# Output product of the later tiles: four of its twelve chunks as three products of rounded parts

## The reference

```python
# 1: attention, 8 heads of 64; only the 32 largest scores of each row count
scores = scale * q @ k.T;  scores[scores < kth] = -1e9
x = softmax(scores) @ v                                  # -> (1152, 512)
# 2: a gated block of width 1536
xn = x / rms(x) * rms_g
x = (silu(xn @ w_gate) * (xn @ w_val)) @ w_out           # -> (1152, 512)
# 3: eight experts; each token goes to its argmax expert, in order of arrival
out[i] = gate_w[i] * (relu(x[i] @ w1[e]) @ w2[e])
```

## Time and profile before

| | |
|---|---|
| median of 3 runs | 632.54 us (632.41 to 633.07) |
| the profiled execution | 632.94 us |
| its span, first to last instruction | 631.1 us |
| TensorE busy | 609.7 us (97%) |
| VectorE busy | 411.0 us (65%; nearly full until 400 us) |
| ScalarE busy | 328.8 us (52%) |
| GpSimd busy | 265.3 us (42%) |
| granted TensorE clock, mean | 0.990 |

### The profile page before, as it was taken

How to read it: one execution, slowest core, us unless ns; L and a number is a source line. 1 busy time by engine, 2 the same in 40 slices (tenths; PEclk the granted TensorE clock), 3 DMA queues, 4 the chain that set the end, 5 groups by cost and what they waited for, 6 DMA issues and landing times.

```text
span 631.1 us, 11127 instructions
## 1 busy us (share of the span) xinstructions
PE 609.7 (97%) x3927; PEld 468.6 (74%) x3927; DVE 411.0 (65%) x912; ACT 328.8 (52%) x713; POOL 265.3 (42%) x375
## 2 busy tenths in 40 slices
PE   7789999999999999999999999999999999999995
PEld 5455765865866766766766766757589999999995
DVE  4999999999898997998998998902011111011110
ACT  4787877767767767767767756744111111111110
POOL 1896875375365464563553654552310110111102
PEclk9799999999999999999999999999999999999998
DMA  9999800000000000000000000000596776767501
GB/s 245 243 379 331 208 19 0 18 18 2 18 18 1 19 18 2 17 18 2 18 17 2 2 18 1 2 17 1 185 391 211 267 264 210 280 204 264 176 2 39
DMA packets 55182, 65.45 MB, mean 104 GB/s; under 512 B 32282, under 2 KB 32282, under 8 KB 55132
## 3 DMA queue, kind: packets, MB, share of 16 engines
q1 hardware_dynamic: 53388, 60.05, 30.0%
q0 software_dynamic: 1744, 4.76, 2.1%
HBM read 52.89 MB, written 12.30 MB: 103 GB/s over the span
## 4 chain that ended last, share of the span: by engine, by line
PE 81%; DVE 14%; issue 3%; ACT 1%; POOL 1%; POOLq 0%; DVEq 0%; ACTq 0%
PE ps L579 13%; PE ps L894 12%; PE ps L877 12%; PE ps L531 7%; PE ps L538 7%; PE ps L532 7%; PE ps L512 6%; PE ps L485 5%; DVE w_top L1418 5%; PE ps L496 4%; DVE m L1414 4%; PE ps L470 4%; DVE w_top L1406 2%; DVE m L1400 1%; PE ps L712 1%
## 5 line engine op out<-in xcount | busy, mean ns | idle before, releaser
L1607 POOL TENSOR_TENSOR s_ring<-s_ring,z_pair 128x576 f32<-128x576 f32 x72 | 100.8, 1421 | 63.1 <-ACT z_pair L1090 63.1
L1418 DVE MATCH_REPLACE8 w_top<-m,w_top 128x576 f32<-128x576 f32 x144 | 105.6, 740 | 0.0
L1414 DVE MAX8 m<-w_top 128x8 f32<-128x576 f32 x144 | 101.4, 744 | 0.0
L579 PE MATMUL ps<-wo_space,hid 128*128 128x512 f32 x216 | 100.5, 593 | 0.0
L531 PE MATMUL ps<-w_parts,x_hi 128*128 128x512 f32 x196 | 81.7, 417 | 0.0
L532 PE MATMUL ps<-w_parts,x_hi 128*128 128x512 f32 x196 | 77.5, 395 | 0.0
L1632 POOL DMA_INDIRECT out_rows<-arena,s_ring x16 | 15.0, 940 | 145.2 <-DVE arena L1442 142.7
L894 PE MATMUL ps<-arena,w_loads 128*128 128x168 f32 x512 | 75.9, 307 | 0.0
L877 PE MATMUL ps<-arena,w_loads 128*128 128x168 f32 x512 | 74.4, 306 | 0.0
L877 PEld LDWEIGHTS ps<-arena,w_loads 128*128 128x128 f32 x512 | 73.3, 190 | 0.3 <-ACT arena L955 0.2
L894 PEld LDWEIGHTS ps<-arena,w_loads 128*128 128x128 f32 x512 | 73.2, 190 | 0.1
(11 more groups left out here) (143 smaller groups left out, 911.6 us busy)
## 6 DMA issues: line engine op xcount, KB each, us to landing
w_loads<-in_moe_w SPq DMA_DIRECT2D x16, 2048.0 KB, 9.0
dispatched_rows<-drow SPq DMA_DIRECT2D x18, 260.0 KB, 6.9
w_loads<-in_moe_w_gate SPq DMA_DIRECT2D x3, 1024.0 KB, 6.2
w_loads<-in_moe_w_val SPq DMA_DIRECT2D x3, 1024.0 KB, 8.5
wo_space<-in_moe_w_out SPq DMA_DIRECT2D x1, 3072.0 KB, 11.3
arena<-dispatched_rows SPq DMA_DIRECT2D x8, 341.2 KB
out_rows<-drow SPq DMA_DIRECT2D x9, 256.0 KB, 5.2
q_space<-in_q SPq DMA_DIRECT2D x8, 256.0 KB, 3.2
```

What stands on the lines that cost most here:

```text
L579: last = mm(out_bank(t), hid[:, c * P:(c + 1) * P], wo_s[:, c, :], start=(c == 0), stop=(c == CF - 1))
L1414: vec.max(m8[:, 2 * (n % 2) + a, i, :], w_top[:, a, :]).then_inc(s["top_step"], 1)
L1418: vec.match_replace(w_top[:, a, :], m8[:, 2 * (n % 2) + a, i, :], w_top[:, a, :], NEG).then_inc(s["top_step"], 1)
L1607: gp.tensor_tensor(row, row, z_pair[:, a, :], ALU.subtract).then_inc(s["lowered"], 1)
```

## The change

The product with `w_out` of tiles 4 to 8 (`PARTED` = 4) takes its chunks 0 to 3 (`PARTS`) as three products of rounded parts; the other eight chunks, and all of tiles 0 to 3, stay as they were. The parts need space: `wo_hi` and `h_hi` lie where the first batch's values were, `wo_lo` over chunks 0 to 3 of `w_out` itself, and `h_lo` over the first 512 columns of `hid`. Those of the weights are made once: ScalarE rounds chunks 0 and 1 at the end of slot 21, GpSimd rounds 2 and 3 in slot 22 and subtracts in slots 22 and 23. Those of `hid` are made by GpSimd for each tile (`part_hidden`) one slot before they are used. `stay_awake`, which multiplies only to keep TensorE occupied, reads four chunks further on.

```diff
+PARTED, PARTS, FINE = 4, 4, 4
...
+        wo_hi = fine(FREE_AT, PARTS * DM).rearrange("p (c d) -> p c d", c=PARTS)
+        wo_lo = fine(OUT_AT, PARTS * DM).rearrange("p (c d) -> p c d", c=PARTS)
+        h_hi, h_lo = fine(FREE_AT + PARTS * DM, PARTS * P), fine(HID_AT, PARTS * P)
...
+            def fine_chunk(t, c):
+
+                hi, lo = h_hi[:, c * P:(c + 1) * P], h_lo[:, c * P:(c + 1) * P]
+                mm(out_bank(t), hi, wo_hi[:, c, :], start=(c == 0), stop=False)
+                mm(out_bank(t), hi, wo_lo[:, c, :], start=False, stop=False)
+                mm(out_bank(t), lo, wo_hi[:, c, :], start=False, stop=False)
+
             def ffn_out(t, i):
...
+                    if t >= PARTED and c < PARTS:
+                        if c == 0:
+                            pe.wait_ge(s["out_lo_set"], 2)
+                            pe.wait_ge(s["h_lo_set"], t - PARTED + 1)
+                        fine_chunk(t, c)
+                        continue
                     last = mm(out_bank(t), hid[:, c * P:(c + 1) * P], wo_s[:, c, :], start=(c == 0), stop=(c == CF - 1))
...
+                    if t == PARTED:
+                        act.wait_ge(s["wo_in"], 16)
+                        act.wait_ge(s["pv_done"], 2 * HP * (MIX + 1))
+                        for c in range(PARTS // 2):
+                            copy(wo_hi[:, c, :], wo_s[:, c, :]).then_inc(s["out_hi_act"], 1)
...
+            def part_hidden(t):
+
+                pool.wait_ge(s["t_free"], use["h0", t] + 1)
+                if t > PARTED:
+                    pool.wait_ge(s["out_full"], t)
+                raw = hid[:, 0:PARTS * P]
+                gp.tensor_copy(h_hi, raw).then_inc(s["h_hi_set"], 1)
+                pool.wait_ge(s["h_hi_set"], t - PARTED + 1)
+                gp.tensor_tensor(h_lo, raw, h_hi, ALU.subtract).then_inc(s["h_lo_set"], 1)
...
+                half = PARTS // 2
+                if due(n, ALPHA, 0) == PARTED:
+                    pool.wait_ge(s["wo_in"], 16)
+                    pool.wait_ge(s["pv_done"], 2 * HP * (MIX + 1))
+                    gp.tensor_copy(wo_hi[:, half:PARTS, :], wo_s[:, half:PARTS, :]).then_inc(s["out_hi_pool"], 1)
+                    pool.wait_ge(s["out_hi_act"], half)
+                    pool.wait_ge(s["out_full"], PARTED)
+                    gp.tensor_tensor(wo_lo[:, 0:half, :], wo_s[:, 0:half, :], wo_hi[:, 0:half, :],
+                                     ALU.subtract).then_inc(s["out_lo_set"], 1)
+                if due(n, ALPHA, 3) == PARTED:
+                    pool.wait_ge(s["out_hi_pool"], 1)
+                    gp.tensor_tensor(wo_lo[:, half:PARTS, :], wo_s[:, half:PARTS, :], wo_hi[:, half:PARTS, :],
+                                     ALU.subtract).then_inc(s["out_lo_set"], 1)
...
                 dense(n, ALPHA)
+                t = due(n, BETA, FINE)
+                if t is not None and t >= PARTED:
+                    part_hidden(t)
```

More of the change, by code:

```diff
@@ L104, in build @@
         GV = CD * FF
+        ARENA = 2 * (HP * S + KC * H * D)
+        OUT_AT, ARENA_AT = 0, CF * DM
+        HID_AT = ARENA_AT + ARENA
         with nc.sbuf_tensor("w_parts", [P, 4 * GV], F32) as w_parts:
@@ L107, in build @@
         w_loads = sb("w_loads", [P, 4 * GV])
+        with nc.sbuf_tensor("out_parts", [P, HID_AT + FF], F32) as out_parts:
+            pass
         wo_space = sb("wo_space", [P, CF * DM])
-        arena = sb("arena", [P, 2 * (HP * S + KC * H * D)])
+        arena = sb("arena", [P, ARENA])
+        hid = sb("hid", [P, FF])
         s_ring = sb("s_ring", [P, SR, 2, S])
@@ L120, in build @@
         gain = sb("gain", [P, CD])
-        hid = sb("hid", [P, FF])
         drow = sb("drow", [P, ROW])
@@ L168, in build, with fine @@
               .rearrange("p (j h d) -> p j h d", j=KC, h=H) for b in range(B)]
+        FREE_AT = ARENA_AT + v0
+        def fine(at, width):
+            return out_parts[:, at:at + width].bitcast(F32R)
+        wo_hi = fine(FREE_AT, PARTS * DM).rearrange("p (c d) -> p c d", c=PARTS)
+        wo_lo = fine(OUT_AT, PARTS * DM).rearrange("p (c d) -> p c d", c=PARTS)
+        h_hi, h_lo = fine(FREE_AT + PARTS * DM, PARTS * P), fine(HID_AT, PARTS * P)
         w1_s = [w_loads[:, a:a + CD * F].rearrange("p (c f) -> p c f", c=CD) for a in (2 * GV, 0)]
@@ L219, in build @@
             "den_step normed col_full col_copied col_turned x_sum pstep rinv_set x_hi_set blk_full tanh_done silu_done val_copied val_done "
-            "first_spots chosen out_full out_copied picked ranked_set lneg_set spot_base lexp_set gate_step row_ready seen_set dispatched last_dispatched most_set "
+            "first_spots chosen out_full out_hi_act out_hi_pool out_lo_set h_hi_set h_lo_set out_copied picked ranked_set lneg_set spot_base lexp_set gate_step row_ready seen_set dispatched last_dispatched most_set "
             "meta_in xs_in0 xs_in1 w1_a w1_b w2_a w2_b xt_half xt_done xt_act xt_vec h_done h_act h_vec "
@@ L598, in stay_awake @@
                 for c in range(count):
-                    mm(blk[1][:, 0:384], ident[:], wo_s[:, c, 0:384], start=True, stop=True)
+                    mm(blk[1][:, 0:384], ident[:], wo_s[:, PARTS + c, 0:384], start=True, stop=True)
             def first_rows(c):
```

## The result

The changed kernel takes 634.90 us, median of 10 runs (632.72 to 636.08), against 632.85 us for the kernel before in 10 runs beside it (632.41 to 634.19). The ratio is 1.0032, with a 95% interval of 1.0022 to 1.0041: 0.32% slower, some 2.0 us, where 2.15 us less were forecast. The profiled execution has a span of 632.7 us. What lies outside the span has changed too: 1.8 us in the runs of the kernel before, 2.1 to 2.3 in those of the changed one, so that 0.3 us of the loss is not between the first and the last instruction. No run here shows where it comes from.

A forecast was written before the change was run, and what follows sets the result against it. TensorE was taken to bound the kernel. Products -3.25 us and a one-time stall of +1.1 gave -2.15, taking the median of 632.54 to 630.4 us; the 8-in-10 range was 628.9 to 632.1.

The forecast's parts named there:

- Bound: Tile stages: TensorE, busy 46.00 of 46.00 us, sets the pace; time off its list comes off the end.
- The products: TensorE, tiles 4 to 8: a chunk takes 0.698 instead of 0.860 us; 20 chunks save 3.25 us.
- the change from one kind to the other: TensorE, chunk 3 to chunk 4, once a tile: taken as 0, at most 0.1 us a tile, 0.5 in all.
- the rival of a gain that is waited away: Tiles: VectorE becomes the pace or savings are waited for before transpositions; 632.35 us, no change; chance 0.13.
- The one-time preparation: Slot 22: GpSimd's subtraction waits for ScalarE's copies, lowering starts 1.55 us late, TensorE stalls 1.1 us (0 to 2.3).
- GpSimd in every tile: `part_hidden` takes GpSimd 1.9 us a tile, 2.6 at most, fits its idle time and costs TensorE 0.
- the slower rival: Slots 24, 28, 32, 36: long `part_hidden` delays lowering and TensorE's transposition; 636.0 us; chance 0.05.
- The last tile and the experts: Tile 8, stage 3: weights come 1.9 us later but have 5.6 us of cover; tile 8 keeps its 0.65 us saving.

The follow-up runs named there:

- swap_rows_first: rows_first with the two one-time subtractions exchanged, so GpSimd subtracts its own chunks first and does not wait for ScalarE: 630.39 us, ratio 0.9953.
- plain_rows_first: rows_first with all parts made and waited for, but the first four chunks of tiles 4 to 8 multiplied at the plain float32 price: 634.25 us, ratio 1.0018.
- late_stream: The kernel before, with the experts' weights asked for only after the last transposition of tile 8's hidden values: 637.74 us, ratio 1.0072.
- rows_first: The changed kernel, with SyncE asking for expert 1's rows ahead of expert 1's second weights instead of behind them: 631.50 us, ratio 0.9979.
- send_first: The changed kernel, with every `part_hidden` behind GpSimd's send of the earlier tile instead of ahead of it: 634.32 us, ratio 1.0022.
- awake: The changed kernel, with three unused matmuls ahead of the transposition of expert 1's rows to keep TensorE busy: 634.48 us, ratio 1.0029.

## Why the prediction was wrong

**Bound.** Right. In the tiles TensorE set the pace, and the time taken off its list arrived at stage 3: 1.76 us of the forecast 2.15, and 2.01 with the 0.25 that the trace had ahead by itself.

**The products.** The price per product was right: the new matmuls of tile 8 start 0.23 us apart, and the change from one kind to the other in the middle of a piece cost nothing that shows. These are rows of TensorE's timeline of the changed kernel: two products of chunk 0, the last product of chunk 3, and the plain chunks behind it:

```profile
447.07 0.39 PE L592 MATMUL ps<-out_parts 128*128 128x512 f32 x1
447.30 0.40 PE L593 MATMUL ps<-out_parts 128*128 128x512 f32 x1
...
449.36 0.39 PE L593 MATMUL ps<-out_parts 128*128 128x512 f32 x1
449.59 1.88 PE L607 MATMUL ps<-wo_space,hid 128*128 128x512 f32 x4
```

By the kernels the term was 2.75 (2.5 by the ratios) instead of 3.25. What is missing is one tile: in slot 36, tile 7, TensorE comes to chunk 4 before ScalarE has copied the hidden values. These are its first part-product, the first plain chunk behind the parts, and the transposition behind the six chunks:

```profile
412.87 0.48 PE L591 MATMUL ps<-out_parts 128*128 128x512 f32 x1
...
416.52 1.98 PE L607 MATMUL ps<-wo_space,hid 128*128 128x512 f32 x4 [0.65 <-ACT hid L983]
418.34 0.60 PE L511 MATMUL ps<-ident,s_ring 128*128 128x128 f32 x4
```

From the first to the last it is 5.47 us, and in the kernel before 5.32 (414.36 to 419.68): tile 7 gains nothing, where tile 4 gains 0.67. In slot 36 the first six chunks follow each other with no scores between them, so the faster four bring TensorE there too early. It is the rival of a gain that is waited away, at one place of the five.

**The one-time preparation.** Right in mechanism and place, and near in size. GpSimd waited 2.60 us for ScalarE's copies, lowering came 1.1 us late (1.36 counted from the values product of slot 21), and TensorE waited before both transpositions of slot 22. The values products of slots 21 and 22, before and in the changed kernel, measure it:

```profile
252.29 1.31 PE L512 MATMUL ps<-pt,arena 128*64 128x128 f32 x20
262.52 1.31 PE L512 MATMUL ps<-pt,arena 128*64 128x128 f32 x20
```

```profile
252.04 1.31 PE L527 MATMUL ps<-pt,arena 128*64 128x128 f32 x20
263.20 1.31 PE L527 MATMUL ps<-pt,arena 128*64 128x128 f32 x20
```

11.16 us instead of 10.23: a stall of 0.93, against 1.1 forecast. In swap_rows_first the distance is 10.22 again (252.31 to 262.53), and the runs put the stall at 1.1. The 1.2 of plain_rows_first holds 0.3 outside the span, which the forecast took as unchanged. The rounding of 128x1024 took 1.05 (taken as 1.1), that of 128x512 0.61 (taken as 0.6).

**GpSimd in every tile.** Right: 1.9 us, no wait of TensorE for its parts anywhere, and the slower rival did not come about. By plain_rows_first a cost in every tile is not there: its span is 0.9 us longer, and the stall of slot 22 alone is 0.93.

**The last tile and the experts: the step that failed.** It says: "Tile 8 therefore keeps its 0.65, and all that TensorE gained shifts the whole of stage 3." I had seen that `part_hidden` of tile 8 holds up the send of tile 7 and with it the weights, and had checked it against the first product alone, with 5.6 us of cover. That cover was real: L905 begins without a wait, and tile 8 did keep its 0.65. But the weights are four transfers of 2 MB from one list, and behind them on the same list are expert 1's rows, which are needed 14.0 us after the first product (479.95 - 465.99 before), not when expert 1 begins. How much those had to spare I did not ask. The trace of before could not have said it as a wait, since there was none. It was to be had from the landing of the fourth load, 476.4, and the place of L860, 479.95: 3.5 us for a transfer that stands behind that load and that took 2.2 in the changed kernel, so some 1.3 to spare. late_stream bears it out: its stream starts 4.4 us later (454.98, less the 1.0 by which its trace is late, against 449.55) and 3.4 of waiting came of it, so about 1 us was there. The change took 2.0 by arriving early and 1.2 by the later landing of the stream, 1.9 more than the 1.3. So in place of the step the runs showed a wait of 1.87 us for expert 1's rows and 1.74 lost behind it, 3.6 in all, where the sum had nothing.

The Trainium skill, in "DMA: Bandwidth & Descriptors", section "Two DMAs through the same engine are not ordered", says that within one queue of one engine descriptors start in order though they need not complete so. The trace agrees as to the starts: the 341 KB asked for at 470.42, while the fourth load was under way, landed at 479.76, 2.2 us behind it, and in rows_first, with one load less ahead, they were not waited for at 478.17.

**The clock.** The prediction reckoned a stall at its length. This one cost 1.87 and then 1.68. The Trainium skill, in "TensorE: Matmul & The Clock Gate", section "What's actually happening", says that the granted clock follows how busy the engine has been of late. The trace agrees in part: the clock fell to 0.50 behind the wait of 1.70 (the change) and to 0.52 behind 3.39 (late_stream), but not behind the two waits of 1.49 and 1.59 in send_first. This is the stage of the send_first kernel in which the wait of 1.59 has just ended, at 449.70 (columns as above, the granted clock third from the end):

```profile
450.00:452.00 2.00, 2.00 (x10) 1.64 (x9) 0.00 (x0) 0.00 (x0) 0.80 (x1) 1.00 0.94 273
```

The clock is 1.00 there, and in the stages behind it. What was lost behind the wait was about 1.7 us both times that the clock fell, whatever the wait, and nothing the other two times. Which stall lowers the clock, these runs do not show.

**Accounts.** -3.25 was forecast for the products, of which about 2.7 came; +1.1 for the preparation, of which 0.93 came; and +3.6 (1.87, 0.06 and 1.68) at a wait and the clock behind it that the sum did not have, and +0.3 outside the span, which it took as unchanged. That is +2.1, and 2.05 was measured. The range ended at 632.1 because its upper end was made of small terms of the tiles; no case in it had a transfer that becomes late, though the text held both halves of one.

## What to carry to other kernels

When a change makes the busiest engine faster *and* delays what starts a stream of transfers, follow the whole list of that stream to its last member, and for each ask when it lands and when it is first needed, not only for the first. A small transfer behind large ones, wanted early, belongs ahead of them. And give a new stall of the matrix engine a second case in the range, with the clock: here 1.7 us more behind two of four such waits, and nothing behind the others.

## What the hardware showed

- A wait of 1.70 us had a granted clock of 0.81, 0.50 and 0.84 behind it, in the stages from 480 to 486 us, and 1.68 us were lost by it; behind a wait of 3.39 us 1.70 were lost; waits of 1.49 and 1.59 us had 1.00 behind them.
- A transfer of 341 KB took 9.34 us behind loads of 2 MB on the same list.
- GpSimd rounds faster than it subtracts: 128x1024 to float32r in 1.05 us, against 2.38 to 2.42 for a subtraction of that size, with the result in float32r too.
- The times of kernels in which TensorE waits for this transfer spread more: 4.2 us between the fastest and the slowest run of awake, 3.4 of the change, against 2.2 of the kernel before in 35 runs, 1.6 of rows_first and 0.5 of swap_rows_first in 5. What makes the stream take longer in one run than in another stays open.
